# Splits of q and k, order of loads and the gate's function in a fused attention and two-MLP kernel

## The chip, the cores and the metric

One Trainium2 chip (trn2), one core of it. The metric is the device time of one execution in microseconds; the kernel before takes 1319.25 us (median of 3 runs, 1316.31 to 1322.47).

## The reference

Attention with capped scores over 4 batches of 12 heads (448 positions, 64 per head), then two MLPs over the 1792 tokens:

```python
scores = scale * np.matmul(q, k.transpose(0, 1, 3, 2))       # scale = 1/8
scores = cap * np.tanh(scores / cap)
attn = np.exp(scores - np.max(scores, axis=-1, keepdims=True))
attn = attn / (np.sum(attn, axis=-1, keepdims=True) + 1e-09)
x = heads_beside_each_other(np.matmul(attn, v))               # 1792 x 768
gate = 1.0 / (1.0 + np.exp(-(x @ w_gate)))                    # 768 x 1536
z = gate * (x @ w_val) @ w_out                                # 1536 x 768
h = z @ w_in                                                  # 768 x 2048
y = (h * np.cos(h)) @ w_out2                                  # 2048 x 768
```

## The kernel before, in words

All matrices are float32. To multiply them in TensorE's faster float32 form, each operand is split in two: hi is the operand rounded to that form, lo the rest. A product of blocks is three matmuls (lines 470 to 472): hi x hi, hi x lo, lo x hi, of 128x128 weights on 128x448 activations.

**Stages.** The kernel first computes the six pairs of heads of batch 0 alone (functions `alone`, 0 to some 128 us of the profile). Then for each batch b it runs four products: the first (gate and value, 12 units), the second (6 units), the third (8 units) and the fourth (6 units), each unit in two halves of 6 or 8 blocks. For b < 3 the heads of batch b+1 run beside them: a pair of heads is cut into four groups of its seven tiles of 128 queries, (0,1), (2,3), (4,5), (6), and there are 24 steps n, one to each half of a unit. Step n computes the scores of group n+4, transposes the probabilities of group n+1, and after every second step multiplies by v. Steps -4 to -1 lie in the last two units of the first product, 0 to 11 in the second, 12 to 23 in the fourth; the third product has none.

**Engines.** TensorE does all products and transposes. ScalarE does tanh (line 642), exp (648), the hi copies of transposed probabilities (668), of x (676), of h (710, 742) and z (714), the sigmoid of the gate (706) and the cosine by a sine (739). VectorE does the row maximum (815), the shift (817), the normalisation (823 to 828), copies of transposed tiles (838), the lo parts (845, 847, 861, 897, 901, 933), the product of gate and value (895), the angle's reduction (923, 926) and the product with the cosine (930). ScalarE's functions lie in tables of which one is loaded at a time; single activations on `warm` at lines 774, 777, 779 and 782 load one ahead of a stage.

**GpSimd** splits: q and k of every pair (`split_qk`, line 320, both heads d = 0, 1), v of batches 1 to 3 (`split_v`) and, in batch 0, all weights (`split_w`: hi by line 315, lo by 318). Its order is written out by hand: all pairs of batch 0, then for every half of a unit the weights of that half, and after certain halves a split of q and k or of v (`split_heads`). A split of a weight half waits until TensorE has ended the same half two units earlier, and TensorE's half waits for its split. `q_hi` is a single buffer; its upper 64 partitions have to be zero, which the split gets by multiplying with `below`, a column that is 0 above and 1 below.

**SyncE** issues nearly all DMAs in one order and waits in that order. In the stage of the heads alone, the load of q and k of pair pr+2 waits for the scores of pair pr, that of v for the product with v that last used the buffer, and the six first weight halves stand between (lines 281 to 289). The split weights go back to memory (`keep`, lines 227 to 232) and are read from there in batches 1 to 3.

The order of the lines that matter most in `alone`'s loads:

```python
for pr in range(PAIRS - 1):
    if pr < PAIRS - 2:
        for d in range(2):
            load_qk(pr + 2, d)
    for d in range(2):
        load_v_alone(pr + 1, d)
    if pr == 1:
        for half in halves[:2 * LO]:
            load_whole(*half)
```

## Time and profile before

| | |
|---|---|
| time, median of 3 runs | 1319.25 us |
| lowest, highest | 1316.31, 1322.47 us |
| profiled execution, its own time | 1325.57 us |
| its span | 1323.8 us |
| mean granted TensorE clock, share of full speed | 0.983 |
| TensorE busy | 1266.4 us (96%) |
| VectorE, ScalarE, GpSimd busy | 716.2, 535.9, 437.3 us |
| DMA | 275.42 MB, mean 208 GB/s |

Busy time is the union of an engine's instructions. Matmuls overlap, so the length of one (some 0.37 us) is longer than the distance from one start to the next (some 0.20 us), and the latter sets the pace. The releaser of a wait is the instruction whose end is seen as having let the waiting one go. The span is a little shorter than the execution's own time, which has what lies around it.

### The profile page before, as it was taken

What the parts mean: (1) busy time and instruction counts of PE and PEld (TensorE: products, weight loads), DVE (VectorE), ACT (ScalarE), POOL (GpSimd) and SP (SyncE); (2) the same over time, 40 slices, a digit from 0 to 9 for tenths busy, and PEclk for the clock granted to TensorE, in tenths of its full rate; (3) what the DMA queues carried; (4) which work ended last, traced back from release to release, by engine and by line L of the source; (5) the groups of instructions that cost most, each with busy time, mean ns of one, the idle gap of its engine ahead of it and who ended that gap; (6) DMA issues with size and microseconds to landing.
All of it is one profiled execution on the core that took longest, in us unless ns stands there. A gap on an engine that the chain in (4) does not pass through costs nothing.

```text
span 1323.8 us, 17368 instructions
## 1 busy us (share of the span) xinstructions
PE 1266.4 (96%) x6328; PEld 1141.5 (86%) x6328; DVE 716.2 (54%) x1340; ACT 535.9 (40%) x1013; POOL 437.3 (33%) x394
## 2 busy tenths in 40 slices
PE   6879998999889999999999999999999999999999
PEld 5546887988789999899999999989999999999998
DVE  6875227898687321588667511388767621113620
ACT  4743116554454111655574211465565411103610
POOL 6271997857986330153301230044300000000000
PEclk8989999999899999999999999999999999999999
DMA  3324888667677676545774576554774556666673
GB/s 90 120 64 155 322 286 309 203 237 244 228 268 288 235 244 222 187 159 171 246 243 149 196 248 216 196 183 154 239 250 156 172 183 214 218 217 218 231 253 108
DMA packets 104292, 275.42 MB, mean 208 GB/s; under 512 B 16656, under 2 KB 24336, under 8 KB 104208
## 3 DMA queue, kind: packets, MB, share of 16 engines
q1 hardware_dynamic: 100608, 268.81, 59.0%
q10 hardware_dynamic: 3600, 5.51, 1.1%
q8 instruction: 51, 0.84, 0.3%
q14 instruction: 33, 0.27, 0.1%
HBM read 215.29 MB, written 58.98 MB: 207 GB/s over the span
## 4 chain that ended last, share of the span: by engine, by line
PE 76%; POOL 7%; DVE 7%; ACT 4%; issue 4%; DMA 1%; SPq 0%; POOLq 0%; ACTq 0%
PE acc L470 21%; PE acc L471 20%; PE acc L472 20%; POOL w_lo L318 3%; PE acc L443 3%; PE t_ps L429 2%; PE acc L460 2%; PE s_ps L402 2%; PE s_ps L403 2%; DVE prob L828 2%; POOL w_hi L315 1%; PE acc L462 1%; PE t_ps L421 1%; ACT prob L648 1%; POOL qk_in L318 1%
## 5 line engine op out<-in xcount | busy, mean ns | idle before, releaser
L470 PE MATMUL acc<-h_hi,w_hi 128*128 128x448 f32 x672 | 252.1, 375 | 0.0
L472 PE MATMUL acc<-h_hi,w_lo 128*128 128x448 f32 x672 | 246.6, 367 | 0.0
L471 PE MATMUL acc<-h_lo,w_hi 128*128 128x448 f32 x672 | 246.5, 367 | 0.0
L470 PE MATMUL acc<-x_hi,w_hi 128*128 128x448 f32 x576 | 213.1, 370 | 3.9 <-POOL w_lo L318 3.3
L471 PE MATMUL acc<-x_lo,w_hi 128*128 128x448 f32 x576 | 211.4, 367 | 0.0
L472 PE MATMUL acc<-x_hi,w_lo 128*128 128x448 f32 x576 | 211.4, 367 | 0.0
L326 POOL TENSOR_SCALAR q_hi<-qk_in_whole,below 128x448 fp32r<-128x448 f32 x47 | 68.8, 1464 | 288.6 <-DMA qk_in_whole<-qk 279.7
L895 DVE TENSOR_TENSOR scratch<-acc,scratch 128x448 f32<-128x448 f32 x48 | 30.0, 624 | 226.7 <-PE acc L472 226.6
L470 PE MATMUL acc<-z_hi,w_hi 128*128 128x448 f32 x384 | 142.7, 372 | 8.3 <-POOL w_lo L318 5.8
L471 PE MATMUL acc<-z_lo,w_hi 128*128 128x448 f32 x384 | 141.9, 370 | 0.0
L472 PE MATMUL acc<-z_hi,w_lo 128*128 128x448 f32 x384 | 141.8, 369 | 0.0
L472 PEld LDWEIGHTS acc<-h_hi,w_lo 128*128 128x128 f32 x672 | 126.8, 189 | 10.4
L471 PEld LDWEIGHTS acc<-h_lo,w_hi 128*128 128x128 f32 x672 | 127.0, 189 | 9.4
L470 PEld LDWEIGHTS acc<-h_hi,w_hi 128*128 128x128 f32 x672 | 126.8, 189 | 9.3
L648 ACT ACTIVATE prob<-prob,shift,cap_abs 128x448 f32<-128x448 f32 x168 | 126.1, 753 | 19.3 <-DVE shift L817 19.0
L318 POOL TENSOR_TENSOR w_lo<-w_lo_whole,w_hi 128x768 fp32r<-128x768 f32 (+1 forms) x64 | 128.6, 2009 | 5.3
L815 DVE TENSOR_REDUCE rowmax<-prob 128x2 f32<-128x896 f32 x96 | 92.5, 963 | 53.7 <-ACT prob L642 53.6
L470 PEld LDWEIGHTS acc<-x_hi,w_hi 128*128 128x128 f32 x576 | 108.6, 189 | 14.6 <-POOL w_lo L318 4.4
L471 PEld LDWEIGHTS acc<-x_lo,w_hi 128*128 128x128 f32 x576 | 108.7, 189 | 9.3 <-issue 0.4
L472 PEld LDWEIGHTS acc<-x_hi,w_lo 128*128 128x128 f32 x576 | 108.7, 189 | 9.1
L828 DVE TENSOR_SCALAR prob<-prob,recip 128x448 f32<-128x448 f32 x168 | 108.5, 681 | 3.4
L710 ACT ACTIVATE h_hi<-scratch 128x448 fp32r<-128x448 f32 x48 | 27.8, 579 | 171.8 <-DVE scratch L895 171.8
(92 smaller groups left out, 2044.0 us busy)
## 6 DMA issues: line engine op xcount, KB each, us to landing
w_lo<-w_pair SPq DMA_DIRECT2D x156, 384.0 KB, 3.8
w_hi<-w_pair SPq DMA_DIRECT2D x156, 384.0 KB, 3.1
qk_in_whole<-qk SPq DMA_DIRECT2D x48, 448.0 KB, 5.4
w_lo_whole<-w SPq DMA_DIRECT2D x52, 384.0 KB, 4.6
w_pair<-w_lo SPq DMA_DIRECT2D x52, 384.0 KB, 4.3
w_pair<-w_hi SPq DMA_DIRECT2D x52, 384.0 KB, 4.8
w_lo<-w_pair SPq DMA_DIRECT2D x36, 512.0 KB, 4.8
w_hi<-w_pair SPq DMA_DIRECT2D x36, 512.0 KB, 3.5
```

Of the source, the lines that this page charges most:

```text
L318: return e.tensor_tensor(out, whole, f32(hi), ALU.subtract)
L326: e.tensor_scalar(q_hi[:, :], q, below[:, 0:1], None, ALU.mult)
L402: e.matmul(to[:, n, 0:S], q, k_hh[pr % 2][d][:, :], start=(d == heads[0]), stop=False)
L443: m = e.matmul(o_alone(pr)[:, 0:S], v_alone[d][:, c, :, :].rearrange("p a d -> p (a d)"), pt_whole[:, c, d * S:(d + 1) * S], start=(d == 0 ...
L470: e.matmul(out[:, 0:S], w_hi[u % HI][:, wb, :], a_hi[:, kb, :], start=first, stop=False)
L471: e.matmul(out[:, 0:S], w_hi[u % HI][:, wb, :], a_lo[:, kb, :], start=False, stop=False)
L472: return e.matmul(out[:, 0:S], w_lo[u % LO][:, wb, :], a_hi[:, kb, :], start=False, stop=last)
L648: e.activation(prob[:, t, :], prob[:, t, :], ACT.Exp, bias=shift[:, t:t + 1], scale=cap_abs[:, 0:1], accum_out=rowsum[:, t:t + 1]).then_in ...
L710: e.activation(h_hi[:, j, :], tmp_b[p], ACT.Copy).then_inc(s_hhi, 1)
L815: e.tensor_reduce(rowmax[:, at], prob[:, at, :], AXIS_X, ALU.max).then_inc(s_max, 1)
L828: e.tensor_scalar(prob[:, t, :], prob[:, t, :], recip[:, t:t + 1], None, ALU.mult).then_inc(s_norm, 1)
L895: e.tensor_tensor(tmp_b[p], acc[2 + p][:, 0:S], tmp_a[p], ALU.mult).then_inc(s_gated, 1)
```

## The change

GpSimd's `split_qk` rounds k first, then only the lower 64 partitions of q (the upper ones stay zero from a memset at the start), and no longer waits for its own last result; for pair 0 the wait for VectorE's use of `q_hi` comes behind the rounding of k. `below` and its two memsets are gone. In the stage of the heads alone a load of v of head 1 stands behind the next load of q and k, and the loads of pairs 6 and 7, the first two of batch 1, are in that stage as well. Their four splits come after the weights of unit 1 instead of beside units 4, 5, 7 and 8. In the third product the splits stand at units 0, 2, 4, 6 (q and k) and 1, 5 (v). The gate is computed as (tanh(x/2) + 1) * value * 0.5, with the half in the two instructions that write h. Exp and normalisation of a group now always come one step behind its tanh; the table with exp and tanh is loaded inside the last unit of the third product, and tanh of step 12's group is done there.

```diff
-PADS = 2 + 3 + 4
+PADS = 2 + 1 + 4
...
             def load_heads(b, stage, j, h):
-                if stage == 1 and h == 0 and j in (0, 2):
+                if stage == 1 and h == 0 and j in (0, 2) and b > 0:
                     for d in range(2):
                         load_qk(first + j // 2, d)
...
             for d in range(2):
                 load_qk(0, d)
-            for d in range(2):
-                load_v_alone(0, d)
+            load_v_alone(0, 0)
             for d in range(2):
                 load_qk(1, d)
-            for pr in range(PAIRS - 1):
-                if pr < PAIRS - 2:
-                    for d in range(2):
-                        load_qk(pr + 2, d)
+            load_v_alone(0, 1)
+            for pr in range(PAIRS):
                 for d in range(2):
-                    load_v_alone(pr + 1, d)
+                    load_qk(pr + 2, d)
+                if pr > 0:
+                    load_v_alone(pr, 1)
+                if pr < PAIRS - 1:
+                    load_v_alone(pr + 1, 0)
...
             def split_qk(pr, d):
                 e.wait_ge(s_qkld[pr % 2][d], 16 * (pr // 2 + 1))
+                rounded(hh[:, :], k).then_inc(s_khi[d], 1)
+                e.wait_ge(s_khi[d], pr + d)
                 if pr == 0:
                     e.wait_ge(s_pad, PADS)
                     e.wait_ge(s_qk[0], 1)
-                e.tensor_scalar(q_hi[:, :], q, below[:, 0:1], None, ALU.mult)
-                rounded(hh[:, :], k).then_inc(s_qkhi[d], 1)
-                e.wait_ge(s_qkhi[d], pr + d)
+                rounded(q_hi[D:P, :], q[D:P, :]).then_inc(s_qhi[d], 1)
+                e.wait_ge(s_qhi[d], pr + d)
                 rest(keys(pr, d), k, hh[:, :])
                 rest(queries(pr, d), q, q_hi[:, :]).then_inc(s_qk[d], 1)
-                e.wait_ge(s_qk[d], pr + 1)
...
             def split_heads(b, stage, j, h):
-                if stage == 1 and h == 1 and j in (4, 5):
-                    split_qk(first, j - 4)
-                if stage == 1 and h == 1 and j in (7, 8):
-                    split_qk(first + 1, j - 7)
+                if stage == 1 and h == 1 and j == 1:
+                    for pr in (first, first + 1):
+                        for d in range(2):
+                            split_qk(pr, d)
...
-                if stage == 3 and h == 1 and j in (2, 3):
-                    split_qk(first + 4, j - 2)
-                if stage == 3 and h == 1 and j in (5, 6):
-                    split_qk(first + 5, j - 5)
-                if stage == 3 and h == 1 and j in (4, 7):
-                    split_v(first + 3, j // 7)
+                if stage == 3 and h == 1 and j in (0, 2):
+                    split_qk(first + 4, j // 2)
+                if stage == 3 and h == 1 and j in (4, 6):
+                    split_qk(first + 5, j // 2 - 2)
+                if stage == 3 and h == 1 and j in (1, 5):
+                    split_v(first + 3, j // 4)
...
 # ScalarE
             def attend(b, n):
-                late = n in (0, 2 * U2)
-                if n > 0 and n + AHEAD - 1 < STEPS and not late:
+                if 0 <= n + AHEAD - 1 < STEPS:
                     exp(group_of(b, n + AHEAD - 1))
-                if n + AHEAD < STEPS:
+                if n + AHEAD < STEPS and n != 2 * U2:
                     tanh(group_of(b, n + AHEAD))
-                if late:
-                    exp(group_of(b, n + AHEAD - 2 if n == 0 else n + AHEAD - 1))
-                if n == -2:
-                    exp(group_of(b, 0))
-                    exp(group_of(b, 1))
                 if 0 <= n + 1 < STEPS:
                     pt_high(group_of(b, n + 1))
-                if n == 0:
-                    exp(group_of(b, AHEAD - 1))
...
-                    e.activation(tmp_a[p], acc[p][:, 0:S], ACT.Sigmoid).then_inc(s_sig, 1)
+                    e.activation(tmp_a[p], acc[p][:, 0:S], ACT.Tanh, scale=0.5).then_inc(s_sig, 1)
...
-                    e.activation(h_hi[:, j, :], tmp_b[p], ACT.Copy).then_inc(s_hhi, 1)
+                    e.activation(h_hi[:, j, :], tmp_b[p], ACT.Copy, scale=0.5).then_inc(s_hhi, 1)
...
 # ScalarE, third product, ahead of the h_hi copies of a unit
+                    if j == U3 - 1:
+                        e.activation(warm[:, :], half_pi[:, :], ACT.Exp)
+                        if heads_beside(b):
+                            tanh(group_of(b, 2 * U2 + AHEAD))
...
-                e.activation(warm[:, :], half_pi[:, :], ACT.Sigmoid)
                 first_product(b)
-                if heads_beside(b):
-                    e.activation(warm[:, :], half_pi[:, :], ACT.Exp)
                 second_product(b)
                 e.activation(warm[:, :], half_pi[:, :], ACT.Sin)
                 third_product(b)
-                if heads_beside(b):
-                    e.activation(warm[:, :], half_pi[:, :], ACT.Exp)
                 fourth_product(b)
...
 # VectorE
-            e.memset(below[0:D, :], 0.0).then_inc(s_pad, 1)
-            e.memset(below[D:P, :], 1.0).then_inc(s_pad, 1)
...
             def attend(b, n):
-                if n == 0:
-                    normalise(group_of(b, AHEAD - 2))
...
-                if n > 0:
-                    if n + AHEAD - 1 < STEPS:
-                        normalise(group_of(b, n + AHEAD - 1))
-                elif n == 0:
-                    normalise(group_of(b, AHEAD - 1))
+                if 0 <= n + AHEAD - 1 < STEPS:
+                    normalise(group_of(b, n + AHEAD - 1))
...
-                        attend(b, step_of(1, j, 0))
-                        if j == U1 - 1:
-                            normalise(group_of(b, 0))
-                            normalise(group_of(b, 1))
-                        attend(b, step_of(1, j, 1))
+                        for h in range(2):
+                            attend(b, step_of(1, j, h))
...
-                    e.tensor_tensor(tmp_b[p], acc[2 + p][:, 0:S], tmp_a[p], ALU.mult).then_inc(s_gated, 1)
+                    e.scalar_tensor_tensor(tmp_b[p], tmp_a[p], 1.0, acc[2 + p][:, 0:S], ALU.add, ALU.mult).then_inc(s_gated, 1)
...
-                    e.tensor_tensor(h_lo[:, j, :], tmp_b[p], f32(h_hi)[:, j, :], ALU.subtract).then_inc(s_h, 1)
+                    e.scalar_tensor_tensor(h_lo[:, j, :], tmp_b[p], 0.5, f32(h_hi)[:, j, :], ALU.mult, ALU.subtract).then_inc(s_h, 1)
```

## Rows read from the trace of the kernel before

**Rows 1.** The page's first part: busy us, share, instructions of each engine.

```profile
PE 1266.4 (96%) x6328; PEld 1141.5 (86%) x6328; DVE 716.2 (54%) x1340; ACT 535.9 (40%) x1013; POOL 437.3 (33%) x394
```

**Rows 2.** TensorE's waits over the span: who waited for whom; us, times, longest.

```profile
PE acc L470 <- POOL w_lo L318: 9.1, 7, 3.6
PE t_ps L429 <- DVE pt_hi L847: 7.9, 7, 2.3
PE acc L402 <- POOL qk_in L318: 5.2, 1, 5.2
PE s_ps L402 <- ACT prob L642: 4.8, 5, 3.5
PE s_ps L402 <- POOL qk_in L318: 3.3, 1, 3.3
...
PE acc L470 <- DVE z_lo L901: 2.5, 1, 2.5
PE t_ps L429 <- DVE prob L828: 1.6, 1, 1.6
```

**Rows 3.** Two stages: length, busy PE, PEld, DVE, ACT, POOL, PEclk, DMA share, GB/s.

```profile
128.00:190.00 62.00, 58.48 (x281) 52.15 (x279) 15.80 (x19) 11.77 (x21) 58.04 (x46) 1.00 0.80 293
...
297.00:370.00 73.00, 64.69 (x294) 57.85 (x293) 54.48 (x68) 34.30 (x61) 63.72 (x48) 0.93 0.72 247
```

**Rows 4.** TensorE's waits after 400 us, all of them.

```profile
PE t_ps L429 <- DVE pt_hi L847: 4.4, 4, 2.3
PE s_ps L402 <- ACT prob L642: 1.2, 4, 0.4
```

**Rows 5.** TensorE in order of time: start, us, instruction, idle before and releaser.

```profile
190.42 0.50 PE L470 MATMUL acc<-x_hi,w_hi 128*128 128x448 f32 x1 [2.32 <-POOL w_lo L318]
190.74 0.56 PE L471 MATMUL acc<-x_lo,w_hi 128*128 128x448 f32 x1
...
229.91 0.55 PE L429 MATMUL t_ps<-ident,prob 128*128 128x128 f32 x3 [1.57 <-DVE pt_hi L847]
...
352.14 0.74 PE L470 MATMUL acc<-z_hi,w_hi 128*128 128x448 f32 x1 [3.61 <-POOL w_lo L318]
...
380.45 0.47 PE L402 MATMUL s_ps<-k_hh,qk_in 128*128 128x448 f32 x1 [3.55 <-ACT prob L642]
```

**Rows 6.** GpSimd in order of time: idle until 130.03, and a split.

```profile
130.03 0.84 POOL L315 TENSOR_SCALAR w_hi<-w_lo_whole 128x768 fp32r<-128x768 f32 x1 [27.18 <-PE acc L472]
...
147.42 1.40 POOL L326 TENSOR_SCALAR q_hi<-qk_in_whole,below 128x448 fp32r<-128x448 f32 x1
148.79 0.56 POOL L315 TENSOR_SCALAR k_hh<-qk_in_whole 128x448 fp32r<-128x448 f32 x1
149.44 1.16 POOL L318 TENSOR_TENSOR qk_in<-qk_in_whole,k_hh 128x448 fp32r<-128x448 f32 x1
```

**Rows 7.** SyncE's issues in order of time.

```profile
46.56 10.74 SPq L212 DMA_DIRECT2D v_hl_whole<-v  x2
57.34 2.99 SPq L225 DMA_DIRECT2D w_lo_whole<-w  x6
60.38 1.61 SPq L207 DMA_DIRECT2D qk_in_whole<-qk  x2
```

**Rows 8.** VectorE in order of time, two normalisations of two tiles.

```profile
46.95 2.46 DVE L828 TENSOR_SCALAR prob<-prob,recip 128x448 f32<-128x448 f32 x2
...
56.95 0.82 DVE L828 TENSOR_SCALAR prob<-prob,recip 128x448 f32<-128x448 f32 x2
```

**Rows 9.** ScalarE and TensorE in order of time, end of batch 1's first product.

```profile
542.16 1.28 ACT L648 ACT_TABLE_LOAD   x1
543.46 0.77 ACT L648 ACTIVATE prob<-prob,shift,cap_abs 128x448 f32<-128x448 f32 x1
...
560.21 0.55 PE L429 MATMUL t_ps<-ident,prob 128*128 128x128 f32 x3 [2.30 <-DVE pt_hi L847]
```

**Rows 10.** ScalarE in order of time, ahead of the fourth product of batch 0.

```profile
376.05 0.67 ACT L739 ACTIVATE scratch<-scratch,half_pi 128x448 f32<-128x448 f32 x1
...
378.00 1.28 ACT L782 ACT_TABLE_LOAD   x1
```

5 lines of the change are left out of this document (2 added, 3 removed).

## The prediction

> **What bounds the kernel now.** I read the page first: TensorE is busy for 96% of the span, no other engine for more than 54% [rows 1]. All matrix work stays, so only the time in which TensorE waits, or runs slowly, can go. The waits of TensorE name its releasers [rows 2]: GpSimd's split of weights 9.1 us, its splits of q and k 5.2 and 3.3, ScalarE's tanh 4.8, VectorE's copies of the transposed probabilities 7.9. The stages come third [rows 3]: between 128 and 190 us GpSimd is busy 58.04 of 62.00 us, between 297 and 370 us 63.72 of 73.00. There it is the bound, and TensorE misses 3.5 and 8.3 us. After 400 us all of TensorE's waits together are 5.6 us [rows 4]: the gain has to come from the first 400 us.
>
> **The price of a wait is more than its length.** TensorE waited 2.32 us at 190.42 for a weight split; the next matmul follows 0.32 us later [rows 5], and the nine after it by some 0.37 each, where 0.20 is its pace elsewhere: 1.5 us more. The same count gives 1.5, 2.4 and 1.2 us behind the waits that end at 229.91, 352.14 and 380.45 [rows 5]; the waits of batches 1 and 2 have no such tail.
>
> **Split of q and k.** Today one is 1.40 (q by the per-partition factor), 0.56 (k), 1.16 and 1.16 us, 4.38 us from start to start [rows 6]. The new q form is the one of k on 64 partitions, which the trace does not show on this engine: I take k's 0.56, by the nearest row; 1.40 is the other end (then a split stays at some 4.4, and part D is worth 3 us less). The extra wait on its own result costs some 0.1 us by the gap of 0.09 between k's end at 149.35 and the subtraction at 149.44. New split: 3.5 us, some 0.9 less, 47 times. What waits behind it is GpSimd's own next split.
>
> **Part A, the heads alone, 0 to 128 us.** (1) k of head 1 is now rounded before the wait for head 0, so its split sheds k's 0.56 and 0.8 of q's: it ends 1.3 us earlier, and TensorE, which waited 3.3 us for it [rows 2], gains that. (2) The load of pair 4 is issued at 60.38, behind a value load that waits for the end of pair 1, and TensorE waits 5.2 us for the split of that data [rows 2], until 73. In the new order it stands behind the value load issued at 46.56 and the six weight loads (2.99 us): issued near 50, landed near 58 after the same 8 us (60.38 to 68.4), split by 65, before TensorE asks at 67 [rows 7]. Gain 5.2. Next in line are VectorE and ScalarE, whose steps are in order already. (3) Against it: the splits of pairs 6 and 7, four of 3.5 us, now run in this stage instead of beside the first product. Where a split meets VectorE's normalisation it stops it: two such instructions took 2.46 us together at 46.95 beside two GpSimd subtractions, 0.82 at 56.95 beside none [rows 8], and TensorE waited 2.7 us. Each split has two subtractions, 2.3 us. From 102.9 to 130.03 GpSimd stands idle today [rows 6], so pair 7 falls into the tail, where blocks of the first product are there to fill; pair 6 falls at 84 to 91 us into steps that count. I charge 2.5 us, one such wait; ends 0 and 10 (four waits). The value loads keep their conditions, and the later loads come earlier: no cost. Two memsets of 0.06 us go from VectorE before it waits for the cap: nothing. **Sum A: 1.3 + 5.2 - 2.5 = 4.0 us.**
>
> The Trainium skill, SBUF — State Buffer, section Who interferes with whom, says that the shared port pair is an exclusive lock and that the loser blocks fully. These rows agree, and it speaks against adding splits here; the rival below is its case.
>
> **Part B, first product of batch 0.** A weight split is 0.83 + 1.84, 2.7 us a half, against 18 matmuls of 0.207, 3.7 us. GpSimd falls behind only by the four splits of q and k, 17.5 us, which are gone. Then nothing is late: GpSimd may work two units ahead. TensorE's waits here, 3.3 of the 3.5 us that it misses [rows 3], go, with the 1.5 behind the longer one. **4.8.** Covering work: none needed.
>
> **Part C, ScalarE and VectorE, end of the first product.** The sigmoid's set has tanh but not exp; of the loads of a batch with heads, four go (lines 774, 648, 706, 777, each 1.28 us) and the load of line 782 moves before the last h_hi copies. Three of the four stand on the chain from step -2 to step 1 in batch 1 (542.16 is the first), 3.85 us, and the orders there put exp and normalise late, which ends in the 2.30 us wait at 560.21 [rows 9]. By the durations of the same rows, the new order in batch 1 runs so: exp(0) and tanh(1) done at 538.2, normalise(0) at 540.8, gate product 541.5 (0.8 later than now), exp(1) and tanh(2) at 544.5, just 0.3 after TensorE's next scores ask; normalise(2) 552, tanh(4) 554.9, VectorE's copies for step 1 done at 557.9 instead of 561.0, as TensorE reaches those transposes. The gate product and the rest of h stay one VectorE instruction each over the same operands, and tanh and the scaled copy one activation each: nothing, covered anyway by the slack of the first ten units. In batch 0 the waits of 1.6 at 217.0 and 1.57 at 229.91 [rows 2, 5] go with 1.5 us of slow matmuls; GpSimd beside it may leave 0.7. **C: 4.0.** The same in batches 1 and 2, 4.4 us of waits, and 1.2 for the tanh [rows 4], of which I count 4.5: **part F, 4.5.**
>
> The Trainium skill, ScalarE: Activation LUTs, section What ACT_TABLE_LOAD costs, gives about 2.66 us for a switch with its drain. By that figure the chain would be 8.0 us shorter per batch. The rows show the next activation at 543.46, 1.30 us after the load's start at 542.16 [rows 9], so no such drain is visible, and the trace decides.
>
> **Part D, third product of batch 0.** The splits move from units 2, 3, 5, 6 to 0, 2, 4, 6, the value splits from 4, 7 to 1, 5. GpSimd's 63.72 us of work, less 4 x 0.9, is 60 us in what would be 65 us for TensorE without its 8.3 [rows 3]: it fits, but only if spread evenly, which is what the new places do. I laid it out with the durations read here (3.1 us a weight half, 4.0 for q and k instead of 5.0, values 1.4): in time up to unit 6, unit 7 some 1.9 us late. So of 5.8 us of waits (9.1 - 3.3) and 2.4 of slow matmuls 2.0 stay: **6.2** (ends 3.5 and 8.2). The loads for the moved splits were issued at 267 us, well before. The 2.5 us for z_lo [rows 2] stay: there VectorE stands behind a weight split that TensorE itself releases.
>
> **Part E, start of the fourth product of batch 0.** TensorE waits 3.55 us at 380.45 for tanh(16) [rows 5], which follows the table load at 378.00, and that the last h_hi copy. In the new order the load follows the last sine (376.05 + 0.67): 1.2 us earlier [rows 10]. Its wait for scores is covered (TensorE ended them near 371). Behind it stand the last two h_hi copies, 2.5 us later, needed only some 12 us after the product's start, and VectorE's next row maximum. **1.2**, ends 0 and 4.7. In batch 3 the extra load falls on idle time.
>
> **Sum.** 4.0 + 4.8 + 4.0 + 6.2 + 1.2 + 4.5 = 24.7 us. The profiled execution took 1325.57 us around a span of 1323.8, 6.3 over the median of the runs, 1319.25; the gain is in waits that every run should have, so 1300.9 for a like profile and 1294.6, say 1294, for the median.
>
> **Rivals.**
> 1. Gains overlap: VectorE and ScalarE, the next in line in the alone stage, in C and in D, take up much of what GpSimd gives back. For it: every step that GpSimd does not touch is chained over both. Against it: steps free of GpSimd run at full pace. A 0, B 4.8, C and F 4, D 3.5, E 0: 12.3 us, 1307.
> 2. The lock, slower: four splits with eight subtractions in the alone stage, each of which may stop VectorE, place 84 to 116 us. If each became a full wait of TensorE, 8 x 2.3 = 18.4 us; with the head start of 1.3 and no gain in C, D, E, but B 4.8 and F 4.5: 18.4 - 1.3 - 4.8 - 4.5, 7.8 us slower, 1327. It decides if over six of the eight cost their whole length; against it, the six pairs split there now cost TensorE only two or three such waits.
> 3. The removed waits are no more than moved: the time of the alone stage is then set by the chain and pair 4's data was just its messenger, and weights come late by GpSimd's port. 3 to 6 us, within the noise: 1315.
>
> **How the numbers follow.** A measurement of this kernel tells about 0.5%, 6.6 us, from no change. The forecast 0.66 (all faster), rival 1 0.20 (nearly all faster), rival 3 0.09, rival 2 0.05. Faster 0.86, same 0.10, slower 0.04. Ends: all at their largest, 8 + 4.8 + 4.7 + 8.2 + 4.7 + 5.6 = 36, 1283; the smallest, -3.5 + 3.3 + 1.5 + 3.5 + 0 + 2 = 6.8, 1312. With 2 in 10 left out: 1283 to 1308.
>
> **What would show it.** TensorE's waits for w_lo nearly gone before 215 us and under 3 us after; no wait for the split of pair 4; q_hi at some 570 ns; two table loads per batch instead of up to six; GpSimd idle beside the first product, waiting only for TensorE; stage one of batch 0 shorter by some 5 us. Wrong it would be if the alone stage ended later than 127 us, or if waits on VectorE's scratch and prob grew by what those on GpSimd shrink.

## The result, and the profile after

The changed kernel takes 1302.62 us (median of 4 runs, 1299.68 to 1304.65). The kernel before, run beside it on the same chip, takes 1320.86 (4 runs, 1316.31 to 1323.63). The ratio is 0.9864, 95% interval 0.9827 to 0.9900: faster, as forecast, and inside the range, but 8.6 us above the forecast of 1294. The profiled executions took 1325.57 and 1304.65 us, 20.9 apart, where the sum of the prediction had 24.7.

The page's first part, of after, beside [rows 1]:

```profile
PE 1261.5 (97%) x6328; PEld 1137.6 (87%) x6328; DVE 718.0 (55%) x1338; ACT 518.8 (40%) x995; POOL 399.5 (31%) x394
```

GpSimd lost 37.8 us of work, ScalarE 17.1, and VectorE nothing. TensorE's waits over the span, of after (who waited for whom; us, times, longest), beside [rows 2]:

```profile
PE acc L443 <- issue: 12.1, 8, 4.5
PE t_ps L429 <- DVE pt_hi L837: 7.0, 5, 4.7
PE acc L470 <- POOL w_lo L318: 3.1, 1, 3.1
...
PE acc L470 <- DVE z_lo L883: 2.7, 1, 2.7
PE s_ps L402 <- ACT prob L642: 2.1, 2, 1.1
...
PE s_ps L402 <- POOL qk_in L318: 1.6, 1, 1.6
```

The waits for weights fell from 9.1 us to 3.1, that for the split of pair 4 (5.2) is gone, that for the first split halved. But the group of pt_hi, the copies of transposed probabilities, went only from 7.9 to 7.0, and its longest wait from 2.3 to 4.7: one new wait has taken the place of several old ones. The same view after 400 us, beside [rows 4], has a single line left:

```profile
PE t_ps L429 <- DVE pt_hi L837: 0.2, 1, 0.2
```

The two stages of [rows 3], of after (length, busy PE, PEld, DVE, ACT, POOL, PEclk, DMA share, GB/s):

```profile
128.00:190.00 62.00, 62.00 (x302) 56.31 (x301) 19.70 (x18) 10.29 (x18) 52.70 (x41) 1.00 0.99 347
...
297.00:370.00 73.00, 64.09 (x310) 57.96 (x309) 63.59 (x76) 42.54 (x78) 65.79 (x45) 0.96 0.80 287
```

In the first TensorE now misses nothing. The second window is no longer the same work, since the third product now ends at 349.5.

**Where the time came from.** Each stretch lies between the starts of two TensorE instructions in the timeline (the 25th block of the first product; the first scores of a step; the first block of a stage). In us, before, after, and what the prediction had:

| stretch | before | after | change | predicted |
|---|---|---|---|---|
| A: start to block 24 of the first product | 134.67 | 128.34 | -6.3 | -4.0 |
| B: to step -4 | 64.83 | 59.52 | -5.3 | -4.8 |
| C: steps -4 to 4 | 48.52 | 44.97 | -3.6 | -4.0 |
| step 4 to the third product | 49.95 | 50.33 | +0.4 | 0 |
| D: third product | 72.22 | 66.38 | -5.8 | -6.2 |
| E: start of the fourth product to step 16 | 34.08 | 37.80 | **+3.7** | -1.2 |
| rest of batch 0 | 53.25 | 53.54 | +0.3 | 0 |
| F: batches 1 and 2 | 614.88 | 610.65 | -4.2 | -4.5 |

Batch 3 is the same to 0.02 us. One term has the wrong sign. That stretch in the timelines of ScalarE, TensorE, VectorE and GpSimd, of after:

```profile
355.01 1.28 ACT L734 ACT_TABLE_LOAD   x1
...
356.42 0.99 ACT L642 ACTIVATE prob<-s_ps,tanh_scale 128x896 f32<-128x896 f32 x1
357.31 1.03 ACT L739 ACTIVATE h_hi<-scratch 128x448 fp32r<-128x448 f32 x2
```

```profile
357.46 0.47 PE L402 MATMUL s_ps<-k_hh,qk_in 128*128 128x448 f32 x1 [1.11 <-ACT prob L642]
...
365.46 0.90 PE L429 MATMUL t_ps<-ident,prob 128*128 128x128 f32 x3 [4.69 <-DVE pt_hi L837]
```

```profile
357.91 3.39 DVE L915 TENSOR_TENSOR h_lo<-scratch,h_hi 128x448 fp32r<-128x448 f32 x2 [2.25 <-ACT h_hi L739]
361.22 1.07 DVE L805 TENSOR_REDUCE rowmax<-prob 128x2 f32<-128x896 f32 x1
362.33 2.32 DVE L807 TENSOR_SCALAR shift<-rowmax,cap_neg 128x2 f32<-128x2 f32 x1
364.56 0.54 DVE L835 TENSOR_TENSOR pt_lo<-t_ps,pt_hi 128x384 fp32r<-128x384 f32 x1
```

```profile
358.15 2.66 POOL L318 TENSOR_TENSOR w_lo<-w_lo_whole,w_hi 128x1024 fp32r<-128x1024 f32 x1
...
362.28 2.34 POOL L318 TENSOR_TENSOR w_lo<-w_lo_whole,w_hi 128x1024 fp32r<-128x1024 f32 x1
```

Table load and tanh now stand ahead of the last two h_hi copies on ScalarE. TensorE gets its tanh earlier, as the term said: it waits 1.11 us for it and not 3.55 [rows 5]. But VectorE idles 2.25 us for those copies; its next instruction in order is h_lo, and that falls on a weight subtraction of GpSimd. It takes 3.39 us; the same two instructions take 1.35 in batch 1 of the kernel before, where GpSimd stands idle:

```profile
686.58 1.35 DVE L933 TENSOR_TENSOR h_lo<-scratch,h_hi 128x448 fp32r<-128x448 f32 x2
```

The row maximum and the shift follow, and the shift, of 2 elements per partition, lasts 2.32 us beside the next subtraction of 2.34. Only then comes pt_low, for which TensorE has waited 4.69 us.

TensorE also runs at half speed behind that wait. These are the profile's rows (columns as in [rows 3]) of that piece of the stretch, and of the one that the kernel before has in its place:

```profile
364.28:371.10 6.82, 5.64 (x19) 4.95 (x20) 6.42 (x18) 5.05 (x11) 0.34 (x1) 0.50 0.26 106
```

```profile
381.88:385.29 3.41, 3.41 (x12) 2.91 (x11) 3.25 (x8) 2.58 (x6) 3.33 (x3) 0.50 1.01 377
```

The granted clock is 0.50 in both, the lower of its two levels (1.2 GHz instead of 2.4), and there matmuls start some 0.37 us apart and not 0.20. Half of TensorE's busy time in such a row is my estimate of what it costs: 2.8 us after, 1.7 before. Waits and low clock of the stretch went from 3.55 + 1.7 to 5.8 + 2.8, which is 3.4 of the 3.7 us.

**The low clock in the other stretches.** By the same estimate, from rows of the same kind, the changes split so: B, waits 3.3 less and low clock 1.7 less (0.50 from 190.73 to 194.15 before, none after); C, 2.2 and 1.7 (231.69 to 235.10 before, none after); D, 2.5 and 2.8 (TensorE busy for 9.0 us at 0.50 before, for 3.4 after). So some 5 of the 10.3 us gained between block 24 and batch 1 are not waits but full clock in place of half.

### The profile page after: what moved, and what is told of

It is laid out like the page before. It is cut to its first block, busy times and chain, and to the rows that moved or that the text cites. A ratio compares the mean times of both kernels' runs of the same rounds, so it can differ in the third digit from the quotient of the medians.

```text
span 1302.9 us, 17315 instructions
## 1 busy us (share of the span) xinstructions
PE 1261.5 (97%) x6328; PEld 1137.6 (87%) x6328; DVE 718.0 (55%) x1338; ACT 518.8 (40%) x995; POOL 399.5 (31%) x394
## 4 chain that ended last, share of the span: by engine, by line
PE 80%; DVE 12%; ACT 4%; issue 4%; DMA 0%; POOL 0%; ACTq 0%; POOLq 0%
PE acc L470 22%; PE acc L472 22%; PE acc L471 22%; PE acc L443 3%; PE t_ps L429 2%; PE acc L460 2%; DVE rowmax L805 2%; PE s_ps L402 2%; PE s_ps L403 2%; DVE prob L818 2%; PE acc L462 1%; PE t_ps L421 1%; DVE pt_lo L835 1%; DVE scratch L908 1%; ACT prob L648 1%
## 5 line engine op out<-in xcount | busy, mean ns | idle before, releaser
L877 DVE SCALAR_TENSOR_TENSOR scratch<-scratch,acc 128x448 f32<-128x448 f32 x48 | 29.8, 621 | 212.8 <-PE acc L472 212.8
L315 POOL TENSOR_SCALAR k_hh<-qk_in_whole 128x448 fp32r<-128x448 f32 x47 | 28.4, 603 | 289.3 <-DMA qk_in_whole<-qk 289.3
L818 DVE TENSOR_SCALAR prob<-prob,recip 128x448 f32<-128x448 f32 x168 | 101.4, 639 | 3.4
```

What stands on the lines that cost most here:

```text
L315: return e.tensor_scalar(out, in_, 1.0, 1.0, ALU.mult, ALU.mult)
L818: e.tensor_scalar(prob[:, t, :], prob[:, t, :], recip[:, t:t + 1], None, ALU.mult).then_inc(s_norm, 1)
L877: e.scalar_tensor_tensor(tmp_b[p], tmp_a[p], 1.0, acc[2 + p][:, 0:S], ALU.add, ALU.mult).then_inc(s_gated, 1)
```

## The experiments

Twelve kernels were run, each on a chip beside the kernel before. Ratios are to that kernel; "us" is a median; stretches are those of the table above. All values by stretch stand in one table at the end of this section.

### The failing term: the order on ScalarE

`tanh_late`: tanh behind the last copies, the table load left ahead of them.

```diff
-                        if heads_beside(b):
-                            tanh(group_of(b, 2 * U2 + AHEAD))
 # behind the h_hi copies
+                    if j == U3 - 1 and heads_beside(b):
+                        tanh(group_of(b, 2 * U2 + AHEAD))
```

> The changed kernel, with tanh of step 12's group moved behind the last two h_hi copies of the third product; the table load stays ahead of them. Theory (order): in the changed kernel VectorE waits 2.25 us for h_hi behind that tanh, so its two h_lo subtractions begin at 357.91, meet GpSimd's weight subtraction and take 3.39 us, and its shift meets the next one; TensorE then waits 4.69 us at 365.46. With tanh behind the copies VectorE starts some 1 us earlier; the wait of 4.69 and the 1.5 us of slow matmuls behind it go for the most part, tanh(16) is 1.1 us later and TensorE's wait for it grows from 1.11 to some 2.2: 2 to 4 us faster than the changed kernel, near 1300. Rival (lock alone): whatever VectorE's start, GpSimd's row of 2.65 us subtractions stops two of its instructions, and a wait of 3 us or more for pt_hi stays at step 13: time within 1 us of the changed kernel's.

Measured: 1298.66 us, ratio 0.9839 (0.9814 to 0.9865). The stretch took 32.22 us and not 37.80; the wait of 4.69 us is gone and this one stands for it, and the granted clock is 1.00 over the whole stretch:

```profile
356.72 0.47 PE L402 MATMUL s_ps<-k_hh,qk_in 128*128 128x448 f32 x1 [2.27 <-ACT prob L642]
```

```profile
347.74:379.96 32.22, 29.30 (x156) 26.34 (x154) 29.26 (x46) 18.80 (x36) 23.17 (x14) 1.00 0.75 280
```

Of the 5.6 us, 2.9 are waits (5.8 to 2.9) and 2.8, by the estimate above, the low clock that this kernel does not have there.

`both_late`: the copies ahead of table load and tanh.

```diff
+                    for h in range(2):
+                        e.wait_ge(s_trig, m + h + 1)
+                        e.activation(h_hi[:, 2 * j + h, :], tmp_b[h], ACT.Copy).then_inc(s_ghi, 1)
                     if j == U3 - 1:
                         e.activation(warm[:, :], half_pi[:, :], ACT.Exp)
 ...
-                    for h in range(2):
-                        e.wait_ge(s_trig, m + h + 1)
-                        e.activation(h_hi[:, 2 * j + h, :], tmp_b[h], ACT.Copy).then_inc(s_ghi, 1)
```

> The changed kernel, with both the table load and tanh of step 12's group behind the last two h_hi copies, as before the change. Theory (order): VectorE's h_lo is as early as before, no wait of 4.69 us at step 13; TensorE waits for tanh(16) some 3.5 us as in the kernel before, with slow matmuls behind: from the start of the fourth product of batch 0 to step 16 34 to 35 us as before the change (34.08) instead of 37.8; 2 to 3 us faster than the changed kernel in all, less 0.5 in each of batches 1 and 2. Rival (lock alone): the stretch stays at 37 us or more.

Measured: 1297.45 us, 0.9826 (0.9798 to 0.9854); stretch 32.78 us, one wait of 2.56 for tanh. In both kernels the copies come first, and in both some 5 us of the stretch return: the cause is the place of tanh ahead of the copies, and with it the order of VectorE's queue, not the table load. The intervals of the ratio overlap with that of the changed kernel (0.9827 to 0.9900), so the time alone would not settle it; the stretch does. In batches 1 and 2 the same stretch costs 29.50 us instead of 29.03: without GpSimd beside it tanh first is the better order.

### The moved splits and the gate, one at a time

`old67`: the splits of pairs 6 and 7 back beside the first product.

```diff
-                if stage == 1 and h == 1 and j == 1:
-                    for pr in (first, first + 1):
-                        for d in range(2):
-                            split_qk(pr, d)
+                if stage == 1 and h == 1 and j in (4, 5):
+                    split_qk(first, j - 4)
+                if stage == 1 and h == 1 and j in (7, 8):
+                    split_qk(first + 1, j - 7)
```

> The changed kernel, with GpSimd's four splits of pairs 6 and 7 back at units 4, 5, 7 and 8 of batch 0's first product. Theory (they cost little in the stage of the heads alone, and cost waits beside the product): TensorE reaches block 24 of the first product 0 to 2 us earlier than the changed kernel's 128.3; between there and step -4 it takes some 3 to 5 us more than 59.5 (splits of 3.5 us instead of 4.4, so a bit less than the 64.8 of before): 2 to 4 us slower. Rival (they stop VectorE where it counts): block 24 over 3 us earlier, and no loss in total.

Measured: 1306.43 us, 0.9889 (0.9865 to 0.9914). The stage alone did not get shorter without the four splits: block 24 at 128.49 against 128.34, and 125.8 to 128.3 in all kernels that have them there. So my charge of 2.5 us for them is not found, nor the 18.4 of rival 2. The first product lost 1.3 us and steps -4 to 0 lost 3.6: a weight wait of 1.75 at 181.94 and a tanh wait of 1.99 at 205.26 came.

`oldgate`: sigmoid, its table loads and the order of exp and normalise as before.

```diff
-                    e.activation(tmp_a[p], acc[p][:, 0:S], ACT.Tanh, scale=0.5).then_inc(s_sig, 1)
+                    e.activation(tmp_a[p], acc[p][:, 0:S], ACT.Sigmoid).then_inc(s_sig, 1)
 ...
+                e.activation(warm[:, :], half_pi[:, :], ACT.Sigmoid)
                 first_product(b)
+                if heads_beside(b):
+                    e.activation(warm[:, :], half_pi[:, :], ACT.Exp)
```

> The changed kernel, with the sigmoid, its table loads, and the old order of exp and normalisation around the end of the first product. Theory: what the stretches step -4 to step 4 lost in batches 0, 1, 2 comes back, 3.5, 3.2 and 2.6 us in the profiles: 8 to 9 us slower than the changed kernel, waits of TensorE for pt_hi of about 2 us at step 1 of each batch. Rival (the stretch got shorter because GpSimd no longer lags and loads come earlier): batch 0 keeps its 3.5 us, only 1 to 3 us slower.

Measured: 1309.6 us, 0.9918 (0.9894 to 0.9942), 7.0 above the changed kernel. The waits for pt_hi, of this kernel, beside the 7.0 of the changed one:

```profile
PE t_ps L429 <- DVE pt_hi L848: 12.4, 11, 4.6
```

Steps 0 to 4 take 26.69 and 26.55 us in batches 1 and 2, as before (27.22, 26.67), where the changed kernel needs 24.23 and 24.11. **In batch 0 the two edits depend on each other**: steps -4 to 4 took 48.52 us before, 48.47 with the old places, 46.60 with the old gate, 44.97 with both changed. The waits alone show it too: 3.4, 3.2, 3.5 and 1.3 us. The rest is mostly the low clock, 0.50 for 3.4 us in the first two kernels and never in the last two. The new gate brings nothing there while GpSimd still splits beside it.

### The order of loads, the form of q, the places in the third product

`old_loads`: v of head 1 again ahead of the next load of q and k; the loads of pairs 6 and 7 stay in the stage.

```diff
-            load_v_alone(0, 0)
+            for d in range(2):
+                load_v_alone(0, d)
 ...
-            load_v_alone(0, 1)
 ...
-                if pr > 0:
-                    load_v_alone(pr, 1)
                 if pr < PAIRS - 1:
-                    load_v_alone(pr + 1, 0)
+                    for d in range(2):
+                        load_v_alone(pr + 1, d)
```

> The changed kernel, with the loads of q, k and v in the stage of the heads alone in the old order (the loads of pairs 6 and 7 stay in that stage, behind the others). Theory: the load of pair 4 is again issued behind the value load that waits for the end of pair 1 and behind the six weight loads, and TensorE waits 3 to 5 us for its split near 65 to 72 us (GpSimd's split is some 2 us shorter than before); block 24 of the first product at 130 to 132 us instead of 126.2 to 128.5: 3 to 5 us slower than the changed kernel. Rival (pair 4 was only the messenger of a chain over VectorE and ScalarE): a wait there, but block 24 within 1.5 us of the changed kernel's, since the waits for the value products shrink by as much.

Measured: 1308.87 us, 0.9906 (0.9876 to 0.9936). Block 24 came at 134.37, 6.0 us later than in the changed kernel and where the kernel before had it (134.67), and the old wait is there again:

```profile
PE acc L401 <- POOL qk_in L317: 5.1, 1, 5.1
```

In the changed kernel SyncE issued that load at 51.94 and not at 60.38 [rows 7], and GpSimd, which had stood idle for that data, began the split at 59.81:

```profile
48.90 3.00 SPq L224 DMA_DIRECT2D w_lo_whole<-w  x6
51.94 1.61 SPq L206 DMA_DIRECT2D qk_in_whole<-qk  x2
```

```profile
59.81 0.56 POOL L315 TENSOR_SCALAR k_hh<-qk_in_whole 128x448 fp32r<-128x448 f32 x1 [14.44 <-DMA qk_in_whole<-qk]
```

So without the new order of loads the other edits bring the stage alone nothing that can be told (0.3 us).

`q_by_factor`: q again times `below` on 128 partitions.

```diff
-                rounded(q_hi[D:P, :], q[D:P, :]).then_inc(s_qhi[d], 1)
+                e.tensor_scalar(q_hi[:, :], q, below[:, 0:1], None, ALU.mult).then_inc(s_qhi[d], 1)
```

> The changed kernel, with q rounded on 128 partitions with the per-partition factor, as before (1.40 us instead of 0.56). Theory: it matters where GpSimd is the bound, in the third product of batch 0: four splits of 0.85 us more, 3.4 us, on top of the 3.12 us that TensorE waits there now, and 0.85 at the very start; elsewhere hidden: 3 to 5 us slower. Rival (subtractions, not the rounding, are what counts, since they stop VectorE): under 1.5 us slower.

Measured: 1305.05 us, 0.9872 (0.9849 to 0.9894), not to be told from the changed kernel. The third product took 71.71 us, 5.3 more, nearly all that part D had gained; its waits for weights:

```profile
PE acc L471 <- POOL w_lo L319: 5.7, 3, 4.6
```

The stretch behind it took 35.09 and not 37.80, so half was given back. Neither theory had both halves. (Kernels with the changed third product take 64.9 to 69.2 us for it, so 2.5 of the 5.3 are outside that scatter; most of the scatter is the granted clock, and with that taken off, below, it is 3.6 to 4.1.) The remainder is pace: batches 1 and 2 took 607.56 us here and 610.65 there (last section). The split of q in the changed kernel is this line of the groups by form; 600 ns is its mean, against 1.40 us in [rows 6]:

```profile
L315 POOL TENSOR_SCALAR q_hi<-qk_in_whole 64x448 fp32r<-64x448 f32 x47 | 28.2, 600 | 4.5 <-DVE qk_in L799 0.7
```

`old_places_third`: the splits in the third product at units 2 to 7, as before.

```diff
-                if stage == 3 and h == 1 and j in (0, 2):
-                    split_qk(first + 4, j // 2)
-                if stage == 3 and h == 1 and j in (4, 6):
-                    split_qk(first + 5, j // 2 - 2)
+                if stage == 3 and h == 1 and j in (2, 3):
+                    split_qk(first + 4, j - 2)
+                if stage == 3 and h == 1 and j in (5, 6):
+                    split_qk(first + 5, j - 5)
```

> The changed kernel, with the splits in the third product back at units 2, 3, 5, 6 (q and k) and 4, 7 (v). Theory: the shorter split alone gives 3.4 us back there, the even spread the rest; TensorE's waits for weights in that product grow from 3.12 to some 5 us, the stretch of the third product of batch 0 from 66.4 to 68 to 70 us (before the change 72.2): 1 to 3 us slower. Rival (the spread is worth nothing, the total of GpSimd's work decides): stretch within 0.7 us of 66.4.

Measured: 1304.42 us, 0.9874 (0.9847 to 0.9902). The third product took 68.41 us, 2.0 more, which lies inside the scatter of that column below; with the stretch behind it, it is 106.7 us against 102.5 to 104.2, which does not. Of part D's 5.8 us the short split is the larger share, the even spread at most some 2 (0.8 to 1.3 with the low clock taken off).

### How long GpSimd's instruction is

If VectorE stands still for one GpSimd instruction at a time, cutting GpSimd's in two should halve the stop. `late_and_cut` is `both_late` with the weight subtractions of the third and fourth products in two:

```diff
-                rest(w_lo[u % LO][:, part, :], whole, hi).then_inc(s_wsplit, 1)
+                lo, half = w_lo[u % LO][:, part, :], BLK[stage] // 2
+                if stage in (3, 4):
+                    rest(lo[:, 0:half, :], whole[:, 0:half, :], hi[:, 0:half, :])
+                    rest(lo[:, half:, :], whole[:, half:, :], hi[:, half:, :]).then_inc(s_wsplit, 1)
+                else:
+                    rest(lo, whole, hi).then_inc(s_wsplit, 1)
```

> The changed kernel with table load and tanh behind the last h_hi copies (1297.45 us when measured), and GpSimd's subtractions for the weights of the third and fourth product each cut in two instructions. Theory (exclusive lock): VectorE waits for one GpSimd instruction at a time, so halves of 1.0 to 1.3 us stop it half as long; TensorE's wait for tanh at the start of batch 0's fourth product falls from 2.56 us to under 2, that for z_lo (2.66) to some 1.5, and the time by 1 to 4 us; GpSimd's own work grows by some 0.1 us for each of 28 cuts. Rival (GpSimd is the bound and the gaps between its instructions are what VectorE gets anyway): the waits for weights in the third product grow by over 1 us and the time is the same or longer.

Measured: 1298.96 us, 0.9826 (0.9805 to 0.9848), the same as `both_late`. The stretch fell by 2.7 to 30.06 us, and the third product grew by 3.3 to 69.61, with 4.6 us of waits for weights. Over the span VectorE's busy time fell by 9.9 us (718.5 to 708.6) and GpSimd's rose by 5.9 (400.1 to 406.0): in the third product, where GpSimd is the bound, VectorE's gain comes with GpSimd's loss. Of the 3.3 us there, 2.1 are waits and 1.7, by the estimate, low clock (0.50 for 6.8 us and not 3.4).

So work had to leave GpSimd in the third product first. `pair5_in_fourth` is `both_late` with the splits of the sixth pair in the fourth product:

```diff
-                if stage == 3 and h == 1 and j in (4, 6):
-                    split_qk(first + 5, j // 2 - 2)
+                if stage == 4 and n in (16, 17):
+                    split_qk(first + 5, n - 16)
```

> The changed kernel with table load and tanh(16) behind the last h_hi copies, and GpSimd's two splits of the sixth pair moved from units 4 and 6 of the third product to the halves of unit 2 of the fourth, where a weight half of some 4 us stands against 6.6 us of TensorE. Theory: the third product's wait for weights (2.3 to 3.1 us, always behind the split of this pair) goes, its stretch in batch 0 falls from 66.3 to 63 to 64 us, the fourth product does not grow by more than 1: 2 to 3.5 us below the 1297.45 us of the kernel with the late tanh alone, 1294 to 1295.5. Rival (the lock: VectorE is now stopped at the start of the fourth product, where its chain sets the pace): stretch to step 16 grows by 2 us or more and the time does not fall.

Measured: 1301.45 us, 0.9858 (0.9834 to 0.9882), 4.0 slower than `both_late`. The third product was down to 62.36 us with no wait for weights, but TensorE then reached the fourth product before VectorE and ScalarE did, and the rival's case came true:

```profile
358.11 0.74 PE L402 MATMUL s_ps<-k_hh,qk_in 128*128 128x448 f32 x1 [6.71 <-ACT prob L642]
```

Ahead of that, one of VectorE's instructions (line 908) took 2.17 us and then 1.48 beside weight subtractions; in batch 1 of the same kernel, with GpSimd idle, it takes 0.62:

```profile
348.85 2.17 DVE L908 SCALAR_TENSOR_TENSOR scratch<-scratch 128x448 f32<-128x448 int32 x1
...
351.58 1.48 DVE L908 SCALAR_TENSOR_TENSOR scratch<-scratch 128x448 f32<-128x448 int32 x1
...
643.20 0.62 DVE L908 SCALAR_TENSOR_TENSOR scratch<-scratch 128x448 f32<-128x448 int32 x1
```

`pair5_and_all_cut` adds to that kernel the cut of `late_and_cut`, now for all four products (this line against the one there):

```diff
-                if stage in (3, 4):
+                if stage in (1, 2, 3, 4):
```

> The same, and all of GpSimd's weight subtractions cut in two instructions. Theory (VectorE waits for one GpSimd instruction at a time, so shorter ones stop it for less): in the stage of the heads alone the wait of 4.5 us near 78 us, beside the four weight subtractions of 1.8 us, falls to 2 or 3; the wait for z_lo (2.66 us) falls; with room in the third product the cuts cost nothing there: 1 to 4 us below the run without cuts. Rival (only the sum of GpSimd's work counts, a cut gives VectorE one stop more): same or slower.

Measured: **1288.71 us, 0.9758 (0.9737 to 0.9779)**, 12.7 below `pair5_in_fourth` by one edit that takes no work from any engine: 7.5 in stretch E, 2.2 between step 4 and the third product, 0.9 in the third product, and 2.6 in the stage alone, where that much is scatter too. Of the 7.5, 5.5 are the wait (6.71 to 1.22) and 2.1 the low clock behind it, which is gone: from 84.5 us on the granted clock never falls in this kernel until its end. The 12.7 are counted from a kernel that is itself 4.0 slower than `both_late`; against `both_late` the move and the cut bring 8.7 together. Page and fourth product's first wait of that kernel:

```profile
PE 1253.9 (98%) x6328; PEld 1134.2 (88%) x6328; DVE 702.0 (55%) x1338; ACT 518.8 (40%) x995; POOL 414.9 (32%) x458
```

```profile
346.79 0.48 PE L407 MATMUL s_ps<-k_hh,qk_in 128*128 128x448 f32 x1 [1.22 <-ACT prob L647]
```

VectorE's busy time fell by 14.1 us (716.1 with one subtraction) for the same instructions, and GpSimd's rose by 13.7, for 64 more. In the stage alone the effect can be seen at one place, where the changed kernel's VectorE stops 2.62 us and TensorE waits 4.52 behind it:

```profile
79.94 2.62 DVE L818 TENSOR_SCALAR prob<-prob,recip 128x448 f32<-128x448 f32 x2
```

```profile
83.26 3.32 PE L443 MATMUL acc<-scratch,v_hl_whole 112*128 112x448 f32 x4 [4.52 <-issue]
```

and in the kernel with the cut 1.98 and 2.59:

```profile
78.29 1.98 DVE L823 TENSOR_SCALAR prob<-prob,recip 128x448 f32<-128x448 f32 x2
```

```profile
80.97 3.25 PE L448 MATMUL acc<-scratch,v_hl_whole 112*128 112x448 f32 x4 [2.59 <-issue]
```

The wait for z_lo stayed at 2.7 us, against what was expected of the cut; why is open.

`light_first_weights`, run once, is the changed kernel with the lo part of the weights of units 0 and 1 written by a rounding instead of a subtraction; it leaves out their true lo part, so it computes something else.

```diff
+                if stage == 1 and j < 2:
+                    rounded(hi, whole).then_inc(s_whi, 1)
+                    e.wait_ge(s_whi, 2 * u + h + 1)
+                    rounded(w_lo[u % LO][:, part, :], whole).then_inc(s_wsplit, 1)
+                    return
```

> The changed kernel; for units 0 and 1 of the first product, whose four halves GpSimd splits beside the heads alone, lo is not computed: it gets the rounded weights by the rounding instruction of 0.83 us instead of the subtraction of 1.83. So the products of these two units are others; all instructions elsewhere stay. Theory (lock): GpSimd's four subtractions at 74.9 to 85.1 us are what stops VectorE; with them 1 us shorter each, TensorE's wait of 4.52 us at 83.26 shrinks by 1.5 us or more, and block 24 comes 1 to 3 us earlier than 126.2 to 128.3. Rival (VectorE's chain is late there of itself): the wait stays at 4 us or more.

Measured: 1298.1 us, a single run. The wait of 4.52 us became one of 2.76 and block 24 came at 123.74, 4.6 us earlier: so at least 1.8 us of that wait were VectorE's stops behind the weight subtractions. The splits of pairs 6 and 7, which this kernel has as well, did not keep it long.

`all_and_qk_cut` cuts the subtractions of q and k as well:

```diff
-                rest(keys(pr, d), k, hh[:, :])
-                rest(queries(pr, d), q, q_hi[:, :]).then_inc(s_qk[d], 1)
+                for lo, whole, hi in ((keys(pr, d), k, hh), (queries(pr, d), q, q_hi)):
+                    for a in (0, S // 2):
+                        m = rest(lo[:, a:a + S // 2], whole[:, a:a + S // 2], hi[:, a:a + S // 2])
+                m.then_inc(s_qk[d], 1)
```

> The version of 1288.71 us (late tanh, sixth pair in the fourth product, weight subtractions in two), and the subtractions of q and k cut in two as well, 0.6 us each instead of 1.13. Theory (one GpSimd instruction at a time stops VectorE): in the stage of the heads alone, where most splits of q and k lie, the waits behind stopped normalisations shrink again, block 24 comes at 123 to 125 us instead of 125.7; some 0.3 us more for GpSimd per split; 1 to 3 us faster in all. Rival (each instruction of GpSimd stops VectorE once, and 0.6 us is near what a stop costs anyway): block 24 and time within 1 us of that version.

Measured: 1286.57 us, 0.9745 (0.9719 to 0.9771). Block 24 came at 123.53 instead of 125.70, the rest of batch 0 is equal within 0.3 us. The 2.2 us are within the scatter of that stage, and the intervals overlap, so this last cut by itself is not shown. It is the fastest version run: 35.7 us under the kernel before in its own comparison, and 16 under the changed one by the medians.

### All of them by stretch

Profiled executions; A to F as above, "D+E" is the third product and the stretch behind it.

| kernel | A | B | C | D | E | D+E | F | span |
|---|---|---|---|---|---|---|---|---|
| before | 134.7 | 64.8 | 48.5 | 72.2 | 34.1 | 106.3 | 614.9 | 1323.8 |
| after | 128.3 | 59.5 | 45.0 | 66.4 | 37.8 | 104.2 | 610.7 | 1302.9 |
| tanh_late | 126.7 | 59.5 | 44.8 | 66.4 | 32.2 | 98.6 | 612.1 | 1296.8 |
| both_late | 126.2 | 58.4 | 45.3 | 66.3 | 32.8 | 99.1 | 611.5 | 1295.4 |
| old67 | 128.5 | 60.8 | 48.5 | 66.3 | 36.8 | 103.1 | 610.5 | 1306.5 |
| oldgate | 127.2 | 58.4 | 46.6 | 67.6 | 36.2 | 103.8 | 616.3 | 1307.4 |
| old_loads | 134.4 | 58.4 | 45.3 | 64.9 | 37.7 | 102.5 | 609.8 | 1305.6 |
| q_by_factor | 129.3 | 58.4 | 45.3 | 71.7 | 35.1 | 106.8 | 607.6 | 1301.9 |
| old_places_third | 126.7 | 58.4 | 45.3 | 68.4 | 38.3 | 106.7 | 611.7 | 1303.5 |
| late_and_cut | 125.8 | 58.4 | 45.3 | 69.6 | 30.1 | 99.7 | 612.1 | 1296.5 |
| pair5_in_fourth | 128.3 | 58.4 | 45.3 | 62.4 | 37.8 | 100.2 | 611.9 | 1299.3 |
| pair5_and_all_cut | 125.7 | 58.4 | 45.3 | 61.4 | 30.3 | 91.8 | 611.1 | 1285.2 |
| light_first_weights | 123.7 | 59.5 | 44.9 | 69.2 | 33.8 | 102.9 | 610.3 | 1296.3 |
| all_and_qk_cut | 123.5 | 58.4 | 45.3 | 61.4 | 30.6 | 92.1 | 612.6 | 1284.8 |

Column A scatters from 125.8 to 128.3 among kernels with the same code in that stage (after, tanh_late, both_late, oldgate, old_places_third, late_and_cut, pair5_in_fourth), column D from 64.9 to 69.2 among those with the same third product (after, tanh_late, both_late, old67, oldgate, old_loads, light_first_weights; four of the seven at 66.3), and D+E from 102.5 to 104.2 among the five of these whose order on ScalarE is the changed one. Differences inside these are not read.

Most of the scatter of column D is the granted clock. Over the third product it is 1.00 in `old_loads` (64.9 us), 0.97 in the four kernels at 66.3 and 66.4, 0.95 in `oldgate` (67.6) and 0.93 in `light_first_weights` (69.2). With half of TensorE's busy time at the low clock taken off, an estimate, all seven come to 64.4 to 64.9 us; `old_places_third` comes to 65.7, the kernel before to 67.7 and `q_by_factor` to 68.5.

## Why the prediction was right, and where not

**A, right in sign, 2.3 us too small.** The earlier load was priced at 5.2 and brought 6.0 (`old_loads`). The split with k first sheds 1.7 us of the first wait (3.3 to 1.6), but with the old loads the stage ends only 0.3 earlier than before, so that gain was taken up. The charge of 2.5 for the splits of pairs 6 and 7 was wrong (`old67`); its end of 0 was in the range. The stop feared there exists, but stands behind the weight subtractions of units 0 and 1 (`light_first_weights`), and in the kernel before a wait of 2.25 us at 99.17 stands beside these too. The ends were summed up with 8 us for A, where its own terms give 1.3 + 5.2 = 6.5 at most, so the low end of the range was some 1.5 us too low.

**B, right.** 5.3 for 4.8. With the old places but the short split the stretch takes 60.84 (`old67`), 4.0 less without any move. But 1.2 of the 4.0 are pace: `old67` runs this stretch at the quicker of two paces (last section), the kernels before and after at the slower. Against kernels of its own pace (58.37) the leaving is worth 2.5, so some 2.8 of the 5.3 had come before it, most likely with the shorter splits. The prediction gave all to the leaving.

**C, right in size, incomplete in cause.** 3.6 for 4.0 in batch 0. I put it down to the tables and orders; the runs show that the gate brings it there only together with the moved splits.

**D, right.** 5.8 for 6.2. One wait of 3.1 us stayed, in front of unit 7 as laid out; priced at 2.0. Waits fell by 2.5 only, and 2.8 are the low clock; that the two add up to the forecast is in part luck. The fallback "part D is worth 3 us less" if q kept its 1.40 us was, against the changed kernel, low: 5.3 in that product, of which 2.5 at least are outside the scatter (3.6 to 4.1 with the low clock taken off), and with the start of the fourth only 2.6.

**E, wrong: the step that failed.** It read "Behind it stand the last two h_hi copies, 2.5 us later, needed only some 12 us after the product's start, and VectorE's next row maximum". It asked when TensorE needs h_hi, and not who else waits for it. VectorE does: h_lo stands ahead of the row maximum, the shift and pt_low in its order, and two of these met a GpSimd subtraction (h_lo 3.39 us, the shift 2.32; the row maximum took its usual 1.07). The 1.2 us came at the tanh (its wait shrank by 2.4), and 4.7 us of a wait for pt_low with it. The term was -1.2, the stretch gave +3.7, and moving tanh behind the copies takes 5.6 us off it. The low clock behind the wait cost 1.1 us more than before on top of that; following the queue would not have shown it. By its own rule, to name what is queued behind a waiting instruction, the term should have walked VectorE's queue to its end. The Trainium skill, SBUF — State Buffer, section Who interferes with whom, has this lock in one sentence (the loser blocks fully); the runs agree, down to a shift of 2 elements that took 2.32 us beside a subtraction of 2.34.

**F, right by two errors.** -4.2 for -4.5. The waits and orders brought 6.7 (steps 0 to 4: 3.0 and 2.6; steps -4 to 0: 0.4; the start of the fourth product: 0.7), and 2.4 went back as slower pace in the second, third and fourth products, 1.15 of it in the third product of batch 1. Why the pace differs is open.

**Its signs.** Most came: q_hi at 0.57 us (the median), two table loads per batch, no wait for the split of pair 4, GpSimd waiting for TensorE alone beside the first product, and the last product of the heads alone ended at 121.4 us instead of 127.7. The waits for w_lo were 3.1 us, not under 3. The sign against it did not: the waits on VectorE's prob and scratch are 4.4 us, 5.0 before.

**The price of a wait.** The prediction adds to some waits a tail of slow matmuls, 1.2 to 2.4 us. These tails are stretches at a granted clock of 0.50, and the price is not one of each wait. Three rows: behind the wait of 3.61 us that ended at 352.14 before, behind the one of 2.32 at 190.42 before, and behind the one of 3.12 at 342.00 after, where the clock stayed whole:

```profile
351.16:357.99 6.83, 5.85 (x16) 5.21 (x17) 3.76 (x3) 1.61 (x3) 6.66 (x6) 0.50 0.76 264
```

```profile
190.73:194.15 3.42, 3.42 (x11) 3.06 (x10) 0.12 (x1) 0.00 (x0) 3.25 (x4) 0.50 0.86 289
```

```profile
342.00:346.00 4.00, 4.00 (x19) 3.66 (x20) 3.24 (x6) 3.25 (x6) 3.92 (x3) 1.00 0.83 292
```

What decides between them is not shown here.

**The table load's price.** After a load at 355.01 the next activation starts at 356.31, 1.30 us on, as in [rows 9]. The Trainium skill, ScalarE: Activation LUTs, section What ACT_TABLE_LOAD costs, gives a drain of about 1.38 us more for a switch of tables. These rows show none, so the estimate of 8.0 us less per batch, worked out from that page, has nothing for it here.

**From the sum to the number.** The sum missed by 3.8 us: E by 4.9, the pace beside steps 4 to 12 and the rest of batch 0 by 0.7, C, D and F by 1.1, with A and B 2.8 the other way. The other 4.9 us of the miss is the step to the median: I took 6.3 us from the profiled time because the profile of before stood so far above its median; the one of after stands only 2.0 above, and 0.6 was rounded away.

**The rivals.** Rival 1, gains that overlap (1307), was nearer to the time than its parts deserve: its A of 0 and D of 3.5 did not come, and the loss sat in E, where VectorE was next in line as it says. Rival 2 had the right mechanism, the lock, in the wrong stage. Rival 3 is out: the order of loads is worth 6 us by itself.

## What to carry to other kernels

Before moving an instruction ahead of others on one engine, ask of each that it passes which other engine's queue stands behind it, and follow that queue to the first thing that TensorE needs; the reader that comes to mind first is not the one that costs. Where VectorE and GpSimd run side by side on the critical path, cut GpSimd's long instructions in two, but only once GpSimd has slack there: alone that cut moved 3 us from one product to the next, with the slack made it was worth 12.7 (8.7 with what making the slack had cost). And when the time of a stretch moves by more than its waits, read its granted clock before looking for another cause: here that was some 5 of the 10.3 us gained behind block 24. Two edits that each remove one of two late arrivals at the same place are worth little singly, so undo each by itself before crediting either.

## What was not expected of the hardware

**The stop goes by instructions.** VectorE's stop lasts until the one GpSimd instruction it meets has ended, whatever its own size: 2.32 us for 128x2 elements (0.23 alone), from 362.33 to 364.65, beside a subtraction from 362.28 to 364.62. Halving GpSimd's weight subtractions took 14.1 us off VectorE's busy time and put 13.7 on GpSimd's.

**Two paces under one clock.** Matmuls of 448 columns start 202.7 ns apart in most stretches and 206.7 in others, both with a granted clock of 1.00. The third product of batch 1, before and after:

```profile
624.26:682.63 58.37, 58.37 (x290) 54.11 (x288) 39.11 (x64) 33.92 (x61) 10.57 (x10) 1.00 0.72 244
```

```profile
604.85:664.37 59.52, 59.52 (x289) 54.05 (x288) 39.95 (x63) 34.06 (x61) 11.48 (x13) 1.00 0.69 242
```

It takes 58.37 to 58.73 us in half of the kernels and 59.52 in the others, and the stretch B 58.37 or 59.52 wherever TensorE has no wait in it. It comes in whole stretches; over batches 1 and 2 it makes up to 3 us between kernels whose code there is the same but for the form of one GpSimd instruction. Its cause is not known.

**The form of a GpSimd operation sets its time more than the partitions.** With a factor read from a column the rounding of q took 1.40 us on 128 partitions; with constants a rounding took 0.56 to 0.60, on 64 partitions (q) and on 128 (k) alike. The factor form on 64 partitions was not run.
